# Attention, gated MLP and soft mixture of experts in one kernel: w_outT's loads in two pairs, fold products in fp32r, the last long block's dispatch behind chunk 4, output columns in three parts

## The chip, the cores and the metric

The kernel runs on one core of one Trainium2 chip. The metric is the device time of one execution in microseconds (us); lower is better. Before the change it is 473.82 us, the median of three runs (473.59 to 474.17).

## What is computed

The reference, cut to what matters:

```python
# attention: batch 4, 8 heads, 768 tokens, head dimension 64, chunks of 32 queries
for c in range(nc):
    q_c = q[:, :, c_start:c_end]                       # 32 queries
    k_full = concatenate([mem_k, k[l_start:r_end]])    # 8 memory keys, 16 to the left, 32, 8 to the right
    scores = scale * q_c @ k_full.T; a = softmax(scores)
    out[:, :, c_start:c_end] = a @ v_full
x = out as [3072 tokens, 512]
h = x @ w_in                                           # 512 to 2048
x = (h * sigmoid(h)) @ w_out                           # 2048 to 512
logits = x @ phi                                       # 32 slots, 4 for each of 8 experts
d = softmax(logits, over the tokens); slot_input = d.T @ x
h = maximum(slot_input[e] @ w1[e], 0); slot_out[e] = h @ w2[e]     # 512 to 1024 to 512
return softmax(logits, over the slots) @ slot_out      # [3072, 512]
```

## The kernel before the change

**Units and blocks.** Attention goes by units of 128 tokens, 24 of them. The MLP goes by seven blocks of 2, 4, 4, 4, 4, 4 and 2 units (256, then 512, then 256 tokens); block 0 and the last block, 6, are the short ones. A block has 16 chunks of 128 hidden features (k from 0 to 15). Each chunk (`pe_mlp`, L287 to L303) is 12 TensorE products: x and w_in are each held as a rounded fp32r part and a rest (`wh`, `wl`; x high and low), and three of the four products of these are taken. ACT casts w_in to `wh` (`act_wh`, L444), POOL and once DVE take the rest (`low_part`, L496). After a chunk, ACT takes the tanh (L404), DVE the gate product g (L505) and a 32x32 transpose of it (L515). Chunk c waits on TensorE for g of chunk c-2.

**Attention of a unit.** TensorE: scores (`pe_scores`, L259). DVE: maximum and subtraction (L476, L478). ACT: exp (L424). DVE: sums and reciprocals (`dve_sums`, L485 to L489). POOL: normalising (L776). TensorE: transposes of the probabilities (L268). ACT and DVE copy these to `pt` (L414). TensorE: product with v (`pe_values`, L282). ACT and DVE write x as its two parts (L434, L494). Units 0 and 1 are done ahead of block 0. The units of the next block are woven between the chunks of the present one: `values_at` and `scores_at` (L48 to L57) say which unit has its values and which its scores in each quarter of a block. In block 0 TensorE transposes the probabilities after chunks 1, 5, 9, 13, and has values of unit 2, 3, 4, 5 and then scores of the next unit after chunks 2, 6, 10, 14.

**Logits without the MLP's output.** w_out and phi are multiplied first: `pe_w2` (L340), 16 products (32 records) of phi with w_outT after chunk 13 of block 0, which need all four w_outT loads; they are transposed after chunk 14 (`pe_w2_T`) and copied to `w2c` (L568). The logits of a block come straight from g (`pe_logits`, L316), in four partition groups. `pe_fold` (L324) sums the groups with a 0/1 matrix `fold`, in fp32: DVE copies them to `part` (L519), the fold follows after chunk 2 of the next block. DVE takes the running maximum (L524, L526), ACT the exp (L439), DVE transposes that to `eB` (L531) and the raw logits to `logits` (L536), and updates the running total (L543).

**Dispatch.** `pe_dispatch` (L336) multiplies these weights with g, so that the sum over tokens is taken of g and not of the MLP's output; DVE adds to `acc` with a decay (L546 to L560). `dispatch_step` (L356) puts it behind chunk 4 of the next block, in the last block behind chunk 7. The fold of block 5 uses the bank `lu_ps`, into which the dispatch writes too; that of block 6 uses `pt_ps`.

**Tail.** After block 6: its own logits, fold and dispatch, with dummy products (`keep_busy`, L899) between them; a sum over groups (L928, L932), the product with w_out (L944), the experts' first layer (L964), its second layer `ffn2` (L652) in two halves of 256 columns, the sums over groups (`slot_outputs`, L660), and the combination of slots by token (`outputs`, L687) in six rounds of 1 MB: three for the left half, run between the tiles of the right half's ffn2, and three after it. ACT and DVE copy each round out of PSUM (L815, L895), SyncE stores it.

**Transfers.** All are issued by SyncE, in one written order with waits (L717 to L756): q/k (0.625 MB) and v (0.5 MB) of each unit, in rings of two; w_in, w_outT, w_out, w1, w2 in pieces of 1 MB. From L609 on, `places` says where each of the 36 late pieces goes and what must be over first: 4 of w_out, 16 of w1, 16 of w2. The order begins with

```python
load_qk(0); load_qk(1); load_v(0); load_w_in(0); load_v(1); load_qk(2); load_w_in(1)
load_qk(3); load_v(2); load_w_in(2); load_v(3); load_w_in(3); load_qk(4); load_v(4)
phi; load_wot(0); load_wot(1); load_qk(5); load_v(5); load_wot(2); load_wot(3); load_qk(6); load_v(6)
```

where load_qk(u) waits for the scores of unit u-2, load_v(u) for the values of unit u-2.

Of the kernel before, what the change touches and what calls it, by code (L numbers as in the profile page):

```python
# [7 lines left out]
QT = 64  # L8
# [3 lines left out]
KC = DM // 128  # L12
# [9 lines left out]
SB = 2  # L22
# [42 lines left out]
def by_token(rounds):  # L65

    import numpy as np
    y = np.empty((NT * QT // 128, 128, DM), rounds.dtype)
    tiles = y.reshape(NT, QT, DM)
    for h in range(2):  # L70
        cols = slice(h * 256, (h + 1) * 256)
        for i, (G0, G1) in enumerate(PAIR):
            got = rounds[h * ROUNDS + i].reshape(128, 2, 4, 256).transpose(1, 2, 0, 3)
            y[4 * G0 - 2:4 * G0 + 2, :, cols] = got[0]
            if G1:
                y[4 * G1 - 2:4 * G1 + 2, :, cols] = got[1]
            else:
                tiles[0:4, :, cols] = got[1][:, 0:64]
                tiles[NT - 4:NT, :, cols] = got[1][:, 64:128]
    return y.reshape(NT * QT, DM)  # L80


def moe_program(nc, qk, v, w_in, w_outT, w_out, phi, w1, w2, out):
# [5 lines left out]
    with ExitStack() as ctx:  # L89
# [21 lines left out]
        eB = at("eB", 4096, [128, TMAX])  # L111
        stats = at("stats", 4608, [128, 8])
# [30 lines left out]
        units.append(at("unit_acc", 1536, [128, HALF_W]))  # L143
        phi_sb = part[:, 0:KC * SLOTS].rearrange("p (k s) -> p k s", k=KC)
# [52 lines left out]
        wh_done, wl_first, wl_done = sem("wh_done"), sem("wl_first"), sem("wl_done")  # L197
# [5 lines left out]
        h_mm, tanh_done, g_done, gb_done = sem("h_mm"), sem("tanh_done"), sem("g_done"), sem("gb_done")  # L203
        l_mm, part_done, fold_mm = sem("l_mm"), sem("part_done"), sem("fold_mm")
# [42 lines left out]
        def pe_scores(pe, u, dispatched=0):  # L247
# [5 lines left out]
            for t in range(2):  # L253
                for c in range(2):
                    for p in range(PAIRS):
                        for h2 in range(2):
                            a, r = place_of(p, h2)
                            at = (2 * t + c) * WIN
                            last = nc.tensor.matmul(s_of(u)[32 * r:32 * r + 32, a, at:at + WIN], q_of(u, t, c, p, h2),  # L259
                                                    k_of(u, t, c, p, h2), start=True, stop=True)  # L260
# [26 lines left out]
        def pe_mlp(pe, b, k):  # L287
# [32 lines left out]
        def pe_fold(pe, b):  # L320
# [3 lines left out]
            nc.tensor.matmul(raw_ps(b)[:, 0:TOKS[b]], fold[:], part[:, 0:TOKS[b]], start=True, stop=True).then_inc(fold_mm, 1)  # L324

        def pe_dispatch(pe, b, units_scored):
            pe.wait_ge(et_done, b + 1)
            pe.wait_ge(raw_kept, 4 * min(b + 1, LAST))
# [27 lines left out]
        def dispatch_step(b):  # L356
            return 7 if b == LAST else 4

        def pe_block(pe, b):
            for k in range(NCH):  # L360
# [6 lines left out]
                if b and k == dispatch_step(b):  # L367
# [7 lines left out]
                if b == 0 and k == 13:  # L375
                    pe_w2(pe)
                if at_pause and scores_at(b, n) is not None:
# [661 lines left out]
```

## Time and profile before the change

| | |
|---|---|
| median of 3 runs | 473.82 us (473.59 to 474.17) |
| the profiled execution | 473.49 us |
| its span | 471.7 us |
| granted TensorE clock, mean | 0.996 of full speed |
| TensorE busy | 451.2 us (96%) |
| weight loads busy | 332.6 us (71%) |
| DVE busy | 274.4 us (58%) |
| ACT busy | 138.7 us (29%) |
| POOL busy | 45.3 us (10%) |
| read and written in HBM | 74.51 MB and 6.29 MB |

All times in the rows below count from the start of the span of the profiled execution. A row of the timeline is one or several like instructions: start, duration, engine, line, what it writes and reads, how many, and in brackets the time for which the engine had stood before it and what ended this. "SPq" is SyncE issuing transfers. The share of a transfer stage is a mean over the core's 16 DMA engines. A TensorE product of fp32 data is two records. Products overlap, so the time from one start to the next is what one costs.

### The profile page before, as it was taken

How to read it: one execution, taken by the hardware profiler on the slowest of the kernel's cores; microseconds unless marked ns; L12 is line 12 of the kernel's file. 1: busy time of each engine (PE TensorE's matmuls, PEld its weight loads, DVE VectorE, ACT ScalarE, POOL GpSimd, SP SyncE). 2: the span in 40 equal slices, each digit the busy share in tenths (PEclk: the TensorE clock that was granted, in tenths of full speed). 3: DMA queues.
4: the chain of work that ended last, by engine and by line, in shares of the span. 5: the costliest groups of instructions: out<-in, count | busy, mean ns of one | idle time of the engine just before them, and what ended most of it. 6: DMA issues, size and time to landing. Idle time of an engine off the chain costs nothing.

```text
span 471.7 us, 12280 instructions
## 1 busy us (share of the span) xinstructions
PE 451.2 (96%) x5460; PEld 332.6 (71%) x5460; DVE 274.4 (58%) x532; ACT 138.7 (29%) x255; POOL 45.3 (10%) x43
## 2 busy tenths in 40 slices
PE   5899999999999999999999999999999999999982
PEld 5799667777876787767777777787677778643551
DVE  5657457765586566766665675568544566551233
ACT  2655233232331322323332323323222121210022
POOL 2476000000000000000000000000000000010000
PEclk9999999999999999999999999999999999999998
DMA  8979222321142153303331231130150479999997
GB/s 330 405 295 375 90 95 96 103 92 50 60 191 55 49 190 101 102 1 102 103 96 51 57 101 60 47 131 1 27 243 0 179 263 406 376 401 423 421 423 323
DMA packets 14308, 81.59 MB, mean 173 GB/s; under 512 B 1584, under 2 KB 1712, under 8 KB 7856
## 3 DMA queue, kind: packets, MB, share of 16 engines
q1 hardware_dynamic: 14256, 80.81, 45.4%
q8 instruction: 43, 0.70, 0.6%
q14 instruction: 9, 0.07, 0.0%
HBM read 74.51 MB, written 6.29 MB: 171 GB/s over the span
## 4 chain that ended last, share of the span: by engine, by line
PE 85%; DMA 6%; DVE 4%; ACT 1%; POOL 1%; issue 1%; DVEq 0%; POOLq 0%
PE h_ps L300 55%; PE o_ps L282 6%; DMA unit<-w 5%; PE lpu_ps L316 5%; PE lpu_ps L336 4%; PE sx_ps L259 3%; PE pt_ps L268 2%; PE sx_ps L336 2%; PE h_ps L964 1%; PE sx_ps L901 1%; POOL sc L776 1%; PE lpu_ps L324 1%; PE h_ps L901 1%; DMA qk_sb<-qk 1%; PE o_ps L944 1%
## 5 line engine op out<-in xcount | busy, mean ns | idle before, releaser
L300 PE MATMUL h_ps<-x_odd,wh 128*128 128x512 f32 x384 | 126.8, 400 | 0.0
L505 DVE SCALAR_TENSOR_TENSOR gT<-gT,h_ps 128x512 f32<-128x512 f32 (+1 forms) x108 | 66.4, 615 | 95.5 <-ACT gT L404 95.0
L404 ACT ACTIVATE gT<-h_ps 128x512 f32<-128x512 f32 (+1 forms) x108 | 58.6, 543 | 185.5 <-PE h_ps L300 184.5
L300 PEld LDWEIGHTS h_ps<-x_odd,wh 128*128 128x128 f32 x384 | 72.1, 188 | 21.4 <-issue 5.1
L300 PE MATMUL h_ps<-x_even,wh 128*128 128x512 f32 x256 | 85.0, 400 | 0.0
L300 PE MATMUL h_ps<-x_odd,wl 128*128 128x512 f32 x192 | 74.9, 390 | 0.0
L515 DVE STREAM_TRANSPOSE gB<-gT 128x512 f32<-128x512 f32 x80 | 56.7, 708 | 2.1 <-issue 0.3
L300 PEld LDWEIGHTS h_ps<-x_even,wh 128*128 128x128 f32 x256 | 48.0, 188 | 12.6 <-issue 2.2
L776 POOL TENSOR_TENSOR sc<-sc,row_stats 128x512 f32<-128x512 f32 x23 | 24.0, 1045 | 280.2 <-DVE row_stats L489 280.2
L300 PE MATMUL h_ps<-x_short,wh 128*128 128x256 f32 x256 | 50.6, 290 | 0.3 <-DVE x_short L494 0.3
L300 PE MATMUL h_ps<-x_even,wl 128*128 128x512 f32 x128 | 49.9, 390 | 0.0
L300 PEld LDWEIGHTS h_ps<-x_short,wh 128*128 128x128 f32 x256 | 41.0, 191 | 5.0 <-issue 3.2
L300 PEld LDWEIGHTS h_ps<-x_odd,wl 128*128 128x128 f32 x192 | 36.1, 188 | 7.4 <-issue 0.5
L300 PE MATMUL h_ps<-x_short,wl 128*128 128x256 f32 x128 | 36.2, 282 | 0.0
L282 PEld LDWEIGHTS o_ps<-pt,v_sb 128*64 128x64 f32 x768 | 24.4, 138 | 8.0 <-issue 7.3
L424 ACT ACTIVATE sc<-sc 128x512 f32<-128x512 f32 x23 | 14.5, 631 | 52.5 <-DVE sc L478 52.4
L282 PE MATMUL o_ps<-pt,v_sb 128*64 128x64 f32 x768 | 27.6, 225 | 0.8 <-DVE pt L414 0.8
L414 ACT COPY pt<-pt_ps 64x512 f32<-64x512 f32 x46 | 26.5, 577 | 6.3 <-PE pt_ps L268 5.8
L300 PEld LDWEIGHTS h_ps<-x_even,wl 128*128 128x128 f32 x128 | 24.1, 188 | 5.1 <-issue 0.5
L259 PEld LDWEIGHTS sx_ps<-qk_sb 64*32 64x32 f32 x1472 | 16.3, 107 | 14.8 <-issue 14.0
L300 PEld LDWEIGHTS h_ps<-x_short,wl 128*128 128x128 f32 x128 | 24.4, 191 | 0.3 <-issue 0.2
L316 PE MATMUL lpu_ps<-gT,w2c 128*32 128x512 f32 (+1 forms) x184 | 22.8, 576 | 0.7 <-DVE w2c L568 0.7
(185 smaller groups left out, 495.4 us busy)
## 6 DMA issues: line engine op xcount, KB each, us to landing
unit<-w SPq DMA_DIRECT2D x31, 1024.0 KB, 9.3
qk_sb<-qk SPq DMA_DIRECT2D x24, 640.0 KB, 5.5
v_sb<-v SPq DMA_DIRECT2D x24, 512.0 KB, 3.6
out<-unit SPq DMA_DIRECT2D x6, 1024.0 KB, 7.4
w_stage<-w_in SPq DMA_DIRECT2D x4, 1024.0 KB, 8.0
wot<-w_outT SPq DMA_DIRECT2D x4, 1024.0 KB, 8.8
unit<-w_out SPq DMA_DIRECT2D x4, 1024.0 KB, 5.4
unit_acc<-w SPq DMA_DIRECT2D x1, 1024.0 KB, 10.2
```

The costliest lines, as they stand in the source:

```text
L259: last = nc.tensor.matmul(s_of(u)[32 * r:32 * r + 32, a, at:at + WIN], q_of(u, t, c, p, h2), k_of(u, t, c, p, h2), start=True, stop=True)
L268: last = nc.tensor.transpose(pt_ps[:, j * 128:(j + 1) * 128], sc_u(u)[:, 2 * j:2 * j + 2, :].rearrange("p c k -> p (c k)"), ident[:])
L282: last = nc.tensor.matmul(o_ps[64 * h2:64 * h2 + 64, at:at + QT], v_sb[:, u % V_RING, t, h * D:(h + 1) * D], pt[:, (2 * a + t) * 4 + r, :] ...
L300: last = nc.tensor.matmul(h_ps[k % 2][:, 0:TOKS[b]], w[:, n, kc, q * 128:(q + 1) * 128], x[:, lo, kc, 0:TOKS[b]], start=(kc == 0 and w is ...
L316: last = nc.tensor.matmul(lg_ps(b)[32 * q:32 * q + 32, 0:TOKS[b]], w2c[:, q, 32 * n:32 * n + 32], gt_of(b, 4 * n + q), start=(n == 0), sto ...
L336: last = nc.tensor.matmul(u_ps[i][32 * c:32 * c + 32, :], eB[32 * i:32 * i + 32, 32 * j:32 * j + 32], gb_groups(b, i, j), start=(r == 0), ...
L404: nc.scalar.activation(gt_of(b, k), h_ps[k % 2][:, 0:TOKS[b]], ACT.Tanh, scale=0.5).then_inc(tanh_done, 1)
L414: copy(pt[half, :, c * CHUNK:(c + 1) * CHUNK], pt_ps[half, :].rearrange("p (j q) -> p j q", q=CHUNK)).then_inc(pt_done, 1)
L424: nc.scalar.activation(sc_u(u)[:], sc_u(u)[:], ACT.Exp, scale=D ** -0.5).then_inc(exp_done, 1)
L505: nc.vector.scalar_tensor_tensor(out=gt_of(b, k), in0=gt_of(b, k), scalar=1.0, in1=h_ps[k % 2][:, 0:TOKS[b]], op0=ALU.add, op1=ALU.mult).t ...
L515: nc.vector.transpose(gb_of(b, k), gt_of(b, k)).then_inc(gb_done, 1)
L776: nc.gpsimd.tensor_tensor(p, p, rinv[:, n % SB, :].unsqueeze(2).to_broadcast([128, 2 * PAIRS, WIN]), ALU.mult).then_inc(p_done, 1)
```

## The change

In the beginning: w_in's first load waits for the first q/k load; load_w_in(3) goes ahead of load_v(3); phi and w_outT's first pair go ahead of load_v(4), and w_outT's second pair ahead of load_v(5). The scores of unit 0 come in two halves, with a maximum of each. DVE has unit 0's sums ahead of unit 1's scores; the normalising of unit 1 is halved between POOL and DVE; the DVE's share of w_in's rest goes to POOL; w_in is cast by column halves and not by row halves, so that two chunks need one half. ACT has cast 1 ahead of unit 1's copy, and exp 2 ahead of cast 2. In block 0 the scores go ahead of the values on TensorE and ahead of x on DVE, the sums ahead of g, the exp one chunk earlier; `pe_w2` goes from chunk 13 to 9, its transposes from 14 to 10.

Folds of blocks 0 to 5: DVE writes the logits as a rounded part and a rest, TensorE takes two fp32r products. Block 5's fold goes to `pt_ps`, and its dispatch goes from chunk 7 to 4 of the last block; the three w1 loads that wait for it go ahead of those that wait for chunk 7.

Tail: fewer dummy products; w_out's four tiles are released one by one; the output columns are finished in three parts of 256, 128 and 128, in seven rounds: three of 1 MB, then 1 and 0.5 MB for either part.

```diff
-ROUNDS = NG // 2
-PAIR = [(1, 2), (3, 4), (5, 0)]
+COLS = [slice(0, 256), slice(256, 384), slice(384, 512)]
+ROUNDS = [(0, (1, 2)), (0, (3, 4)), (0, (5, 0)), (1, (1, 2, 3, 4)), (1, (5, 0)), (2, (1, 2, 3, 4)), (2, (5, 0))]
+DISPATCH_STEP = 4
-W_LOW_BEFORE = {2: (0,), 3: (2, 3), 4: (4, 5), 5: (6, 7)}
+W_LOW_BEFORE = {2: (0, 1), 3: (2, 3), 4: (4, 5), 5: (6, 7)}
...
         def raw_ps(b):
-            return pt_ps if b == LAST else lu_ps
+            return pt_ps if b >= LAST - 1 else lu_ps
...
         def pe_probs_T(pe, u):
             pe.wait_ge(p_done, u + 1)
+            if u == 1:
+                pe.wait_ge(p_half, 1)
...
-            if b == 0 and q == 0:
-                if n == 0:
-                    pe.wait_ge(wl_first, 1)
-                pe.wait_ge(wl_done, 2 * n + 1)
+            if b == 0 and q % 2 == 0:
+                pe.wait_ge(wl_done, 2 * n + q // 2 + 1)
...
+            if b == LAST - 1:
+                pe.wait_ge(pt_done, 2 * NUN)
+            if b == LAST:
+                pe.wait_ge(raw_kept, 4 * LAST)
...
+            pe.wait_ge(fold_rounded, 1)
+            nc.tensor.matmul(raw_ps(b)[:, 0:TOKS[b]], fold_r[:], part_hi[:, 0:TOKS[b]], start=True, stop=False)
+            nc.tensor.matmul(raw_ps(b)[:, 0:TOKS[b]], fold_r[:], part_lo[:, 0:TOKS[b]], start=False, stop=True).then_inc(fold_mm, 1)
...
+                if b == 0 and at_pause:
+                    pe_scores(pe, scores_at(0, n))
                 if at_pause and values_at(b, n) is not None:
                     pe_values(pe, values_at(b, n))
...
-                if b == 0 and k == 13:
+                if b == 0 and k == 9:
                     pe_w2(pe)
...
+            nc.vector.tensor_copy(part_hi[:, 0:TOKS[b]], lg_ps(b)[:, 0:TOKS[b]]).then_inc(parthi_done, 1)
+            dve.wait_ge(parthi_done, b + 1)
+            if b:
+                dve.wait_ge(u_mm, b)
+            nc.vector.tensor_tensor(part_lo[:, 0:TOKS[b]], lg_ps(b)[:, 0:TOKS[b]], part_hi[:, 0:TOKS[b]].bitcast(fp32),
+                                    ALU.subtract).then_inc(part_done, 1)
...
-                if b and k % 4 == pause(b) + 1 and scores_at(b, n) is not None:
+                if k % 4 == pause(b) + 1 and scores_at(b, n) is not None:
                     dve_sums(dve, scores_at(b, n))
...
-            if n == 1:
+            if n == 0:
                 places += [(i, u_mm, NB - 1) for i in (9, 10, 11)]
...
-        places += [(places[u][0], si_mm, 1) for u in range(NF)]
+        places += [(places[u][0], si_mm, u + 1) for u in range(NF)]
...
             load_v(0)
+            sp.wait_ge(qk_in[0], 16)
             load_w_in(0)
...
             load_w_in(2)
+            load_w_in(3)
             load_v(3)
-            load_w_in(3)
             load_qk(4)
-            load_v(4)
             sp.dma_start(phi_sb, phi).then_inc(phi_in, 16)
             load_wot(0)
             load_wot(1)
+            load_v(4)
             load_qk(5)
-            load_v(5)
             load_wot(2)
             load_wot(3)
+            load_v(5)
...
             act_wh(act, 0)
             act_x(act, 0)
+            act_wh(act, 1)
             act_pt(act, 1)
-            act_wh(act, 1)
             act_x(act, 1)
+            act_exp(act, 2)
             act_wh(act, 2)
-            act_exp(act, 2)
...
-            dve_scores(dve, 0)
-            dve_scores(dve, 1)
-            dve_sums(dve, 0)
-            dve_sums(dve, 1)
-            pt_half(dve, nc.vector.tensor_copy, 0, 1)
...
+            dve_first_scores(dve)
+            dve_sums(dve, 0)
+            dve_scores(dve, 1)
+            pt_half(dve, nc.vector.tensor_copy, 0, 1)
+            dve_sums(dve, 1)
+            normalise(nc.vector, dve, 1, 4, 2 * PAIRS, p_half)
             dve_x(dve, 0)
             pt_half(dve, nc.vector.tensor_copy, 1, 1)
-            low_part(nc.vector, dve, 1, wl_first)
+            dve_scores(dve, 2)
             dve_x(dve, 1)
-            dve_scores(dve, 2)
...
-            for e in range(E):
-                ffn2(pe, 1, e)
-                if e == 0:
-                    slot_outputs(pe, 0)
-                if e % 2 and e // 2 < ROUNDS:
-                    outputs(pe, 0, e // 2)
-            keep_busy(3, ex_ps)
-            slot_outputs(pe, 1)
-            keep_busy(4, ex_ps)
-            for i in range(ROUNDS):
-                outputs(pe, 1, i)
+            for part in (1, 2):
+                for e in range(E):
+                    ffn2(pe, part, e)
+                    if e == 0:
+                        slot_outputs(pe, part - 1)
+                    if e % 2 and part == 1 and e < 6:
+                        outputs(pe, e // 2)
+                    if part == 2 and e in (1, 3):
+                        outputs(pe, 3 + e // 2)
+            keep_busy(3, s_ps)
+            slot_outputs(pe, 2)
+            keep_busy(4, s_ps)
+            outputs(pe, 5)
+            outputs(pe, 6)
```

## Rows read from the trace of the kernel before

**Rows 1.** Busy time by stage: from:to, length, PE, PEld, DVE, ACT, POOL, clock, DMA share, GB/s

```profile
196.00:260.00 64.00, 64.00 (x758) 47.79 (x758) 41.23 (x73) 19.86 (x36) 4.18 (x4) 1.00 0.26 77
...
384.00:386.00 2.00, 1.76 (x39) 1.39 (x42) 1.64 (x5) 0.59 (x2) 0.00 (x0) 1.00 0.58 246
...
462.00:464.00 2.00, 1.15 (x16) 0.77 (x16) 1.84 (x4) 1.42 (x4) 0.00 (x0) 1.00 0.57 238
468.00:470.00 2.00, 0.00 (x0) 0.00 (x0) 0.00 (x0) 0.00 (x0) 0.00 (x0) 0.50 1.06 442
```

**Rows 2.** Timeline of the beginning: units 0 and 1, first MLP chunk, unit 2

```profile
7.58 0.63 ACT L424 ACTIVATE sc<-sc 128x512 f32<-128x512 f32 x1 [5.56 <-DVE sc L478]
...
9.23 0.68 DVE L485 TENSOR_REDUCE row_stats<-sc 128x8 f32<-128x512 f32 x1
...
10.50 1.04 POOL L776 TENSOR_TENSOR sc<-sc,row_stats 128x512 f32<-128x512 f32 x1 [7.26 <-DVE row_stats L489]
...
19.01 0.39 PE L300 MATMUL h_ps<-x_short,wh 128*128 128x256 f32 x1 [0.31 <-DVE x_short L494]
...
23.28 0.66 PE L268 MATMUL pt_ps<-ident,sc 128*128 128x128 f32 x4 [1.14 <-POOL sc L776]
```

**Rows 3.** Timeline of block 0: transposes of units 3 and 5, the first logits

```profile
32.14 0.66 PE L268 MATMUL pt_ps<-ident,sc 128*128 128x128 f32 x4 [0.41 <-POOL sc L776]
...
50.07 0.66 PE L268 MATMUL pt_ps<-ident,sc 128*128 128x128 f32 x4 [0.60 <-POOL sc L776]
...
60.56 1.50 PE L316 MATMUL lpu_ps<-gT,w2c 128*32 128x256 f32 x24 [0.75 <-DVE w2c L568]
```

**Rows 4.** The chain that ended last: start, duration, engine, tile, line, records

```profile
50.73 3.57 PE lpu_ps L346 x32
...
134.44 0.86 PE lpu_ps L324 x2
135.30 5.49 PE h_ps L300 x24
```

**Rows 5.** Issues of q/k 4 and of w_outT 2 and 3, us to landing

```profile
18.49 0.43 SPq L704 DMA_DIRECT2D qk_sb<-qk  x1
...
qk_sb<-qk SPq DMA_DIRECT2D x1, 640.0 KB, 9.1
...
35.72 0.92 SPq L715 DMA_DIRECT2D wot<-w_outT  x2
...
wot<-w_outT SPq DMA_DIRECT2D x1, 1024.0 KB, 8.0
```

**Rows 6.** Timeline of block 2: the running total, then the dispatch

```profile
139.43 0.22 DVE L543 SCALAR_TENSOR_TENSOR stats<-stats 128x1 f32<-128x1 f32 x1
...
141.16 0.61 PE L336 MATMUL lpu_ps<-gB,eB 32*32 32x512 f32 x1
```

**Rows 7.** The tail: issues and chunks in time, each issue's us to landing

```profile
385.25 0.33 SPq L743 DMA_DIRECT2D unit<-w  x1
...
389.91 3.07 PE h_ps L300 x24
...
403.16 0.33 SPq L743 DMA_DIRECT2D unit<-w  x1
...
unit<-w SPq DMA_DIRECT2D x1, 1024.0 KB, 7.1
...
431.71 24.93 DMA unit<-w
...
462.45 0.33 SPq L755 DMA_DIRECT2D out<-unit  x1
...
out<-unit SPq DMA_DIRECT2D x1, 1024.0 KB, 4.0
...
465.09 0.33 SPq L755 DMA_DIRECT2D out<-unit  x1
...
out<-unit SPq DMA_DIRECT2D x1, 1024.0 KB, 6.2
```

More of the change, by code:

```diff
@@ L62, in pause, with width, words, by_token @@
     return 2 if b == 0 else 1
-def by_token(rounds):
+def width(r):
+    return COLS[ROUNDS[r][0]].stop - COLS[ROUNDS[r][0]].start
+def words(r):
+    return 4 * len(ROUNDS[r][1]) * width(r)
+def by_token(stored):
     import numpy as np
-    y = np.empty((NT * QT // 128, 128, DM), rounds.dtype)
+    y = np.empty((NT * QT // 128, 128, DM), stored.dtype)
     tiles = y.reshape(NT, QT, DM)
[L70 to L76, printed above, removed]
-            else:
-                tiles[0:4, :, cols] = got[1][:, 0:64]
-                tiles[NT - 4:NT, :, cols] = got[1][:, 64:128]
+    for r, (part, groups) in enumerate(ROUNDS):
+        sixth, at = STORED[r]
+        cols = COLS[part]
+        got = stored[sixth][:, at:at + words(r)].reshape(128, len(groups), 4, width(r)).transpose(1, 2, 0, 3)
+        for rows, G in zip(got, groups):
+            if G:
+                y[4 * G - 2:4 * G + 2, :, cols] = rows
+            else:
+                tiles[0:4, :, cols] = rows[:, 0:64]
+                tiles[NT - 4:NT, :, cols] = rows[:, 64:128]
     return y.reshape(NT * QT, DM)
@@ L252, in pe_scores @@
                 pe.wait_ge(acc_done, 4 * dispatched - 1)
[L253 to L260, printed above, removed]
+            for ps in (range(0, 2), range(2, 4)) if u == 0 else (range(PAIRS),):
+                if ps[0]:
+                    last.then_inc(s_first, 1)
+                for t, c, p, h2 in itertools.product(range(2), range(2), ps, range(2)):
+                    a, r = place_of(p, h2)
+                    at = (2 * t + c) * WIN
+                    last = nc.tensor.matmul(s_of(u)[32 * r:32 * r + 32, a, at:at + WIN], q_of(u, t, c, p, h2),
+                                            k_of(u, t, c, p, h2), start=True, stop=True)
             last.then_inc(s_mm, 1)
@@ L621, in moe_program @@
         sources += [w1[4 * q + j, i] for q in range(2) for i in range(2) for j in range(4)]
-        sources += [w2[h, e] for h in range(2) for e in range(E)]
+        sources += [w2[i] for i in range(2 * E)]
         out_u = [units[places[NF + u][0]] for u in range(NU - own - NF, 2 * E)]
@@ L669, in out_ps, with slot_outputs @@
-        def out_ps(r):
-            return out_sets[1 if r > ROUNDS and (r - ROUNDS) % 2 else 0]
-        def outputs(pe, h, i):
-            r = ROUNDS * h + i
-            if i == 0:
-                pe.wait_ge(so_done, h + 1)
-                if h == 0:
-                    pe.wait_ge(cT_done, 1)
-            before = r if r <= ROUNDS else r - 1
-            if before:
-                pe.wait_ge(out_act, 2 * before)
-                pe.wait_ge(out_dve, 2 * before)
-            for gg in range(2):
+        def slot_outputs(pe, part):
+            n = COLS[part].stop - COLS[part].start
+            pe.wait_ge(so_cp, part + 1)
+            nc.tensor.matmul(so_ps[part][:, 0:n], fold[:], so_in[:, COLS[part]], start=True, stop=True).then_inc(so_mm, 1)
@@ new lines, in dve_slot_outputs, with outputs @@
+        def dve_slot_outputs(dve, part):
+            n = COLS[part].stop - COLS[part].start
+            dve.wait_ge(ffn2_mm, part + 1)
+            nc.vector.tensor_copy(so_in[:, COLS[part]], ffn2_ps[part][:, 0:n]).then_inc(so_cp, 1)
+            dve.wait_ge(so_mm, part + 1)
+            nc.vector.tensor_copy(so4[:, COLS[part]], so_ps[part][:, 0:n]).then_inc(so_done, 1)
+        def out_ps(r):
+            return out_sets[r == NR - 1]
+        def outputs(pe, r):
+            part, groups = ROUNDS[r]
+            n = width(r)
+            if r == 0:
+                pe.wait_ge(cT_done, 1)
+            pe.wait_ge(so_done, part + 1)
+            others = r - 1 if r == NR - 1 else r
+            if others:
+                pe.wait_ge(out_act, 2 * others)
+                pe.wait_ge(out_dve, 2 * others)
+            for i, G in enumerate(groups):
@@ L782, in _ @@
         def _(act):
+            act.wait_ge(const_set, 5)
+            nc.scalar.copy(fold_r[:], fold[:]).then_inc(fold_rounded, 1)
             act_exp(act, 0)
```

163 lines of the change are left out of this document (91 added, 72 removed).

## Prediction

> **What bounds the kernel now.** I read the table of stages first. In blocks 1 to 5 TensorE is busy without a gap (64.00 of 64.00 us) and DVE is at 41.23 [rows 1]: there only TensorE's own work counts. In block 0 TensorE stands once per attention unit, waiting for the normalised probabilities: 1.14 us before unit 2, 0.41 before unit 3 (the gap before unit 4 is like it), 0.60 before unit 5, and 0.75 for w2c at the end [rows 2, 3]. From chunk 15 of the last block on the transfers bound. The load issued behind that chunk, at 403.16, lands 7.1 us later, at 410.3, and the last load, 18 loads on, at 431.71 + 24.93 = 456.64: 2.57 us each. The last of the six stores is down 14.65 us after that (465.09 + 6.2 = 471.3): 2.44 us each [rows 7]. So one transfer of 1 MB follows another to the end, and only an earlier start of this queue, or fewer bytes, would shorten it. The change moves the same bytes.
>
> **The parts, against the profiled execution.** Its time is 473.49 us (span 471.7); the median of the three runs is 0.33 us above it.
>
> A. *First MLP chunk.* Unit 0's exp starts at 7.58 and takes 0.63, but its sums start only at 9.23, behind unit 1's scores, and the normalising follows at 10.50 [rows 2]. With sums 0 ahead they start at about 8.0 (0.3 us of it from the scores in halves), so unit 0 gains 1.2 us. Unit 1's chain now starts behind sums 0, which costs about 1.2; halving its normalising between DVE and POOL gives back up to half of 1.04, and its wait behind unit 0 on TensorE was 1.1 anyway. On ACT the cast of w_in's second half now stands ahead of unit 1's copy, and with the scores of unit 2 on DVE x of unit 1 comes out 0.8 us earlier: chunk 0 starts at 18.2, not 19.0. Gain 0.8; ends 0 (DVE's order gives nothing) and 1.2. w_in's first load waits for the first q/k load; I cost that at nothing, since the two transfers ahead of it still keep the queue full until it could start.
>
> B. *Unit 2.* Exp 2 now comes ahead of a cast, its scores ahead of x of unit 1. Its normalising is done about 20.4, and TensorE gets there at 18.2 + 3.0 = 21.2 instead of 22.1. The 1.14 us stall [rows 2] goes: 1.1 (0.6 to 1.1).
>
> C. *Rounds of units 3 and 4.* Scores go ahead of values, which takes about 1.1 us out of the loop; but the sums now stand ahead of g of the same chunk, and two chunks later TensorE waits for that g, by my count 0.3 of the 0.5 gained. I take 0.3 of each round's gap, 0.6 for both (0 to 0.9). TensorE then comes to the transposes of unit 4 at 41.0 - 0.8 - 1.1 - 0.6 = 38.5.
>
> D. *w2's product at chunk 9 instead of 13.* Its work, 3.57 us [rows 4], is only moved. But it needs all four w_outT loads, at 38.5 + 0.5 = 39.0. Now the third of them lands at 35.72 + 8.0 = 43.7 [rows 5], and the fourth one transfer later, at 46.2. The new order issues the first two before unit 2's values, at about 19, and the last two at about 26, behind v 4 and q/k 5. The queue is full until q/k 4 lands, at 18.49 + 9.1 = 27.6 [rows 5]. Behind that come, by size, 5.1 transfers of 1 MB: four of w_outT, v 4 (0.5) and q/k 5 (0.625). At 2.57 us [rows 7] these are 13.2, and I add an estimated 0.7 for phi's many small rows: 41.5. So TensorE, which had no wait here, stands 2.5 us: cost 2.5. Ends: 0 (all in time) and 7.2 (landing as late as now, 46.2). I take 2.5: the spacing of queued transfers is the nearest row.
>
> E. *Rest of block 0.* w2c is ready long before the logits, so the 0.75 goes; of the 0.60 before unit 5 [rows 3] a part stays, behind g as in C, and the transposing of w2 moves with its copy on DVE. Gain 1.1 (0.6 to 1.4).
>
> Block 0 together: 0.8 + 1.1 + 0.6 - 2.5 + 1.1 = 1.1 us.
>
> F. *Folds.* A fold of 512 columns in two fp32 passes takes 0.86; 24 products of fp32r take 5.49, 0.23 each [rows 4]. Two of them are 0.46: 0.40 less. Four such folds lie in blocks 2 to 5, one of 256 columns in block 1 (0.2): 1.8 us, all on TensorE's path. The second DVE operation (0.7) sits in front of the transposes of e and of the raw logits; what follows these on DVE, the running total, starts at 139.43 while the dispatch starts at 141.16 [rows 6]: 1.7 us of slack for 0.7, and 0.4 for TensorE's earlier coming, so nothing. The fifth 512 fold, in block 6, has chunks half as long ahead of it, and DVE's second operation eats a part: counted in G. Ends 1.2 and 2.0.
>
> G. *Tail.* The dispatch of block 5 ends about 384.1 instead of 389.9 (after it 24 products begin at 389.91), and the three loads that hang on it now go ahead of the pair issued at 385.25 [rows 7]. Before that pair the queue has a hole: the DMA share is 0.58 in 384 to 386 [rows 1]. With loads issued at 384.1 the queue runs about 1.2 us earlier. But the load behind chunk 15 cannot start before that chunk ends, and this moves only by the fold's 0.3; the 7.1 us that the load now takes are 3.1 more than the 4.0 of a store that finds the queue free (462.45) [rows 7], so it still stands in a queue, and what the queue gains counts. Net 1.2; ends 0.3 and 2.5. Fewer dummy products, si's four separate releases and DVE's earlier adding to acc save time on TensorE, but none on the queue, which is still full when their loads come: nothing.
>
> H. *Three parts at the end.* Only 1.5 of 6 MB of stores are left after the last load's outputs instead of 3. By the mean share of the DMA engines (0.57 in 462 to 464 [rows 1], and the slice before is like it) some 1.7 us between 460 and 464 are empty and could be filled. The Trainium skill (DMA: Bandwidth & Descriptors, Queues, rings and completion order) says that one copy is split over up to 16 engines, each of which consumes its own ring in order: then a lagging engine sets the landing, and idle ones cannot help it. By the mean share the sum would be 1.7 us better, by that rule nothing. The landings decide for me: six stores in 14.65 us are the full pace, with no hole [rows 7]. So 0 (up to 1.7). The extra 128 small weight loads, the seventh store and the pairs of experts per load lie under the transfers: nothing, and 0.5 if that cover were gone.
>
> Sum: 1.1 + 1.8 + 1.2 = 4.1 us; 473.5 becomes 469.4, and from the median 473.8 becomes **469.7**.
>
> **Rivals.** *w_outT in time.* If the transfers go faster than the spacings say, D is nothing: 467.2. Against it: 13 us of queued bytes behind the landing at 27.6. For it: the two ends of a transfer's pace, 2.44 and 2.57, differ by only 0.7 over five, so it takes a TensorE later than 38.5 at unit 4 too. Chance 0.2.
>
> *The end is filled.* The mean share is right, H gives 1.7: 468.0. For it: the share of 0.57; against it, the pace of the stores. Chance 0.2.
>
> *The queue does not start earlier.* The loads behind chunk 15 set it again, G is 0.3: 470.6. Chance 0.14.
>
> *Slower: w_outT lands as late as now.* The place is w2's product at chunk 9. If the fourth load lands at 46.2, the wait is 7.2 instead of 2.5: 474.4. It also leaves TensorE idle so long that its clock may fall, as at the end, where its last products end before 464 and the granted clock is 0.50 in 468 to 470, the 1.2 GHz level [rows 1]. The Trainium skill (TensorE: Matmul & The Clock Gate, What's actually happening) has the same: an idle array is gated to half rate until it has been busy again. Every us of product work at that level costs one more; with 3 of them the time is 477. It decides from a wait of 2.5 + 4.1 = 6.6 us, a landing at 45.6. Against it: nothing in the new order holds the last two issues beyond unit 2's values. Chance 0.06.
>
> The forecast itself has 0.4. A measurement of this kernel can tell about 0.2% (0.95 us) from no change. Faster by more, below 472.9: 0.90, all cases but the slow one, less 0.04 for a wait in D of over 5.5 us, which gives no change: 0.04; slower: 0.06. The range reaches from both good rivals together (467.2 - 1.2) to D at 5 us: 466.0 to 472.3.
>
> **What would show it.** Chunk 0 of block 0 at about 18.2; no gap before unit 2; a wait for w_outT of about 2.5 us in the first w2 product near 39; block 1's first chunk 1.1 us earlier; the folds at 0.46; block 5's dispatch right behind chunk 4 of the last block; stores still 2.45 us apart to the end. I am wrong if TensorE waits for g or the halved unit 1 longer than counted, if w_outT is there, or if the last load lands less than 14.5 us before the end.

## Result, and the profile after

The changed kernel takes 471.09 us (median of 19 runs, 469.67 to 473.03). The kernel before, beside it on the same chip, takes 473.9 us (19 runs, 472.92 to 474.93). The ratio is 0.9936, 95% interval 0.9925 to 0.9947: faster by 0.64%, where 469.7 us was forecast with a range from 466.0 to 472.3. The profiled execution takes 471.36 us with a span of 469.4, so 2.3 us less than the one before (471.7); the forecast's sum was 4.1. One execution of experiment 2, which took 734.23 us at a granted clock of 0.561, is left out of its median as a slow one.

The table of stages of the kernel after, with the columns of [rows 1]:

```profile
196.00:260.00 64.00, 64.00 (x761) 48.21 (x760) 42.08 (x75) 20.23 (x37) 4.18 (x4) 1.00 0.26 80
384.00:386.00 2.00, 2.00 (x20) 1.91 (x17) 1.86 (x5) 0.19 (x2) 0.00 (x0) 1.00 0.97 406
462.00:464.00 2.00, 0.85 (x32) 0.65 (x24) 1.53 (x3) 1.53 (x4) 0.00 (x0) 1.00 0.38 143
468.00:470.00 2.00, 0.00 (x0) 0.00 (x0) 0.00 (x0) 0.00 (x0) 0.00 (x0) 0.50 0.23 90
```

The middle is as before. The transfers' queue is full at 384 (0.97, was 0.58), as G wanted, but between 462 and 464 it is emptier than before (0.38, was 0.57). The hole near the end was there before too and has moved with the rest: over the whole hole the mean shares leave 1.7 us of 460 to 464 empty before, and 1.9 us of 461 to 465 after.

The beginning and block 0 of the kernel after, from the timeline, the lines that answer to [rows 2, 3]:

```profile
8.43 0.69 DVE L526 TENSOR_REDUCE row_stats<-sc 128x8 f32<-128x512 f32 x1 [0.70 <-ACT sc L453]
9.71 1.04 POOL L536 TENSOR_TENSOR sc<-sc,row_stats 128x512 f32<-128x512 f32 x1 [6.48 <-DVE row_stats L530]
13.39 0.42 DVE L536 TENSOR_TENSOR sc_first<-sc_first,row_stats 128x256 f32<-128x256 f32 x1
13.43 0.85 POOL L536 TENSOR_TENSOR sc_first<-sc_first,row_stats 128x256 f32<-128x256 f32 x1 [2.68 <-DVE row_stats L530]
18.46 0.38 PE L321 MATMUL h_ps<-x_short,wh 128*128 128x256 f32 x1 [0.32 <-DVE x_short L542]
21.43 0.60 PE L291 MATMUL pt_ps<-ident,sc 128*128 128x128 f32 x4
38.42 0.60 PE L291 MATMUL pt_ps<-ident,sc 128*128 128x128 f32 x4
40.28 1.05 PE L376 MATMUL lpu_ps<-wot,part 128*32 128x512 f32 x2 [0.28 <-DMA wot<-w_outT]
42.75 3.62 PE L376 MATMUL lpu_ps<-wot,part 128*32 128x512 f32 x26 [1.42 <-DMA wot<-w_outT]
60.50 1.50 PE L337 MATMUL lpu_ps<-gT,w2c 128*32 128x256 f32 x24
```

Chunk 0 starts at 18.46 (was 19.01), the waits for the probabilities are gone (2.6 us in all before), and unit 4's transposes stand at 38.42, where the forecast had 38.5. Then TensorE is in w2's product from 38.95 to 46.37, 7.42 us for 3.57 of work [rows 4]: 3.85 us of waiting, at a product that did not wait before. The chain of waits tells how much of the gain it takes (start, duration, what):

```profile
26.99 15.71 DMA wot<-w_outT
42.75 3.62 PE lpu_ps L376 x26
...
62.00 2.96 PE h_ps L321 x12
...
322.70 0.23 PE lpu_ps L353
322.92 0.23 PE lpu_ps L354
...
389.20 1.70 PE h_ps L321 x12
...
397.98 3.07 PE h_ps L321 x24
...
455.99 1.22 PE lpu_ps L710 x38
457.22 1.06 issue
458.28 1.03 PE lpu_ps L710 x26
```

Block 1's first chunk stands at 62.00, 0.06 us earlier than before (62.06): block 0's gains are all given back. The last 24 products of the MLP, chunks 14 and 15 of the last block, start at 397.98 (before 400.06), the last store has landed at 468.98 (471.31). So by stage: block 0 gains 0.06, blocks 1 to 6 up to those products gain 2.02 (338.00 becomes 335.98), and the tail, from those products to the last store, gains 0.25 (71.25 becomes 71.00). In the chain of the tail a transfer no longer stands, as it did before with 24.93 us [rows 7]; products, copies out of PSUM and 1.06 us of "issue" do.

### The profile page after: what moved, and what is told of

Its sections match the earlier page's. It is cut to its first block, busy times and chain, and to the rows that moved or that the text cites. A ratio compares the mean times of both kernels' runs of the same rounds, so it can differ in the third digit from the quotient of the medians.

```text
span 469.4 us, 12642 instructions
## 1 busy us (share of the span) xinstructions
PE 451.4 (96%) x5626; PEld 336.0 (72%) x5626; DVE 277.5 (59%) x544; ACT 139.0 (30%) x258; POOL 47.4 (10%) x44
## 4 chain that ended last, share of the span: by engine, by line
PE 88%; DMA 6%; DVE 3%; issue 1%; ACT 0%; SPq 0%; DVEq 0%
PE h_ps L321 54%; PE o_ps L305 5%; PE lpu_ps L337 5%; PE sx_ps L280 4%; PE lpu_ps L366 4%; DMA wot<-w_outT 3%; DMA qk_sb<-qk 3%; PE lpu_ps L710 2%; PE sx_ps L366 2%; PE pt_ps L291 2%; PE h_ps L1024 2%; DVE unit L955 1%; PE h_ps L745 1%; PE sx_ps L961 1%; PE o_ps L1004 1%
## 5 line engine op out<-in xcount | busy, mean ns | idle before, releaser
L280 PEld LDWEIGHTS sx_ps<-qk_sb 64*32 64x32 f32 x1472 | 16.6, 107 | 15.2 <-issue 13.8
```

## The experiments

"At 11" below is the changed kernel with w2's product two chunks later, "after" the changed kernel itself, and "run 5" is experiment 5. Readings of the profiles, in us of the span. The landings are those of the trace's completion records; where two are given, they are the first and the last of the 16 DMA engines. "Product" is the start of the last 26 records of w2's product (at 11: of all 32; before: of all 32 too), "chunk 14" that of the last 24 products of the MLP (chunks 14 and 15 of the last block), "experts" the end of the last expert's product.

```
                        product  block 1  chunk 14  last load        experts  last store  chunk 14 to last store
before                   50.73    62.06    400.06   453.62 456.64    457.75   471.31      71.25
after                    42.75    62.00    397.98   450.76 452.88    459.31   468.98      71.00
w2 at 11                 43.76    57.69    393.66   445.88 448.29    455.40   465.07      71.41
fp32 folds               42.41    61.67    399.89   452.94 456.86    461.51   471.53      71.64
two halves               41.33    60.58    396.56   449.38 453.12    455.09   471.03      74.47
dispatch at 7            42.31    61.55    397.06   450.48 453.32    458.32   467.99      70.93
at 11, round 4 later                       393.87   446.78 449.01    455.58   466.83      72.96
at 11, two halves                 57.77    393.76   445.99 449.04    450.15   465.62      71.86
at 11, dispatch at 7              57.93    393.58   446.43 450.09    455.32   464.99      71.41
at 11, shifted                             394.31   447.27 450.14    458.09   467.74      73.43
at 11, round 4 last               57.69    393.80   446.41 449.47    454.46   465.70      71.90
unit 1 whole             42.86    62.12    398.10   451.34 453.71    459.65   469.31      71.21
scores 0 whole           41.48    60.76    396.87   449.40 452.54    458.21   467.87      71.00
sums 0 late              42.06    61.32    397.42   450.30 453.09    458.89   468.55      71.13
```

**1. w2's product behind chunk 11.**

The same in TensorE's order and in DVE's:

```diff
-if b == 0 and k == 9:
+if b == 0 and k == 11:
...
-if b == 0 and k == 10:
+if b == 0 and k == 12:
```

> w2's product moves from chunk 9 to 11 of block 0 (its transposes to 12), nothing else. Theory: at chunk 9 TensorE stands about 3.8 us for w_outT (product from 38.95 to 46.37 in the changed kernel, 3.57 of it work), and at chunk 11 it would come at about 43.8, after the last landing at 42.7: no wait, block 1's first chunk near 58.5 instead of 62.0, time 471.1 - 3.5 = 467.6. Rival: the wait only stands in for one that follows anyway (w2c late, attention of unit 5 late): block 1 starts at 61 to 62, time 470 to 471.

467.54 us (6 runs), ratio to before 0.9879 (0.9858 to 0.9901). The chain:

```profile
40.34 0.79 PE sx_ps L280 x53
...
43.83 3.57 PE lpu_ps L376 x32
...
57.69 2.96 PE h_ps L321 x12
```

The product takes its 3.57 us in one piece and block 1 starts 4.31 us earlier than after; the medians of the two differ by 3.6 us. Of the 4.31, 3.85 are the wait and 0.12 an earlier chunk 0 (18.34); the remaining 0.34 is not broken down. The rival, that another wait takes its place, falls. That the landing itself sets block 1's start shows in the seven profiles with the product at 9: from the product's last 26 records to block 1 it is 19.24 to 19.28 us in each, while the start itself moves between 60.58 and 62.12 with the landing.

**2. fp32 folds.** All folds again one fp32 product of `part`, DVE's rounding and subtraction left out.

```diff
-nc.tensor.matmul(raw_ps(b)[:, 0:TOKS[b]], fold_r[:], part_hi[:, 0:TOKS[b]], start=True, stop=False)
-nc.tensor.matmul(raw_ps(b)[:, 0:TOKS[b]], fold_r[:], part_lo[:, 0:TOKS[b]], start=False, stop=True).then_inc(fold_mm, 1)
+nc.tensor.matmul(raw_ps(b)[:, 0:TOKS[b]], fold[:], part[:, 0:TOKS[b]], start=True, stop=True).then_inc(fold_mm, 1)
```

> The folds of blocks 0 to 5 are fp32 again and DVE writes one copy; order and banks stay as changed. Theory: TensorE's path gives back 0.4 us for each of five long folds and 0.2 for the short one, 2.2 us: 473.3. Rival: DVE's second operation and its waits cost as much as the faster product gains, then 471.1 to 471.6.

472.91 us (11 runs), ratio 0.9989 (0.9974 to 1.0003). Blocks 1 to 6 take 338.22 instead of 335.98: the folds are worth 2.24 us, and are nearly all that the change as it stands brings.

**3. Two halves.** COLS, ROUNDS and the order behind the second ffn as before.

```diff
-COLS = [slice(0, 256), slice(256, 384), slice(384, 512)]
+COLS = [slice(0, 256), slice(256, 512)]
```

> Output columns in two halves again (six rounds of 1 MB, w2 laid out in halves), all else as changed. Theory: in the changed kernel the end hangs on TensorE and the copies out of PSUM (last load down at 452.9, last store 16.1 us later, where the queue alone needs 14.7); with halves the last store comes 14.7 us after the last load again: 469.6. Rival: the three parts did fill the queue at the end, and halves cost up to 1.7 more: 472.8.

469.99 us (10 runs), ratio 0.9939 (0.9919 to 0.9958), against 0.9936 (0.9925 to 0.9947) of the three parts: no difference that can be told. Its profiled execution is its slowest (473.42, mean clock 0.987), so its 74.47 us of tail are not its usual ones; the other runs lie between 469.26 and 472.13. TensorE waits 2.42 us for the last load in it, the granted clock is 0.50 from 452.81 to 456.22, and the last 16 records of the experts take 1.93 us where they took 1.07 before. The theory's 469.6 holds as a number, the rival's 472.8 does not: three parts bring nothing over two halves. The theory's mechanism, a last store 14.7 us behind the last load, is not what this profile shows (17.9).

**4. Dispatch of block 5 behind chunk 7**, DVE's adding to acc and the three loads with it.

```diff
-if b and k == DISPATCH_STEP:
+if b and k == (7 if b == LAST else DISPATCH_STEP):
```

> Block 5's dispatch behind chunk 7 of the last block again, its three loads behind chunk 7's pair; all else as changed. Theory: the queue starts 1.2 to 1.5 us later and the last load lands at about 454.4, but the end hangs on TensorE and the copies, and TensorE loses the stall behind DVE's adding to acc (0.5): 470.6 to 471.2. Rival: the queue still sets the end, then 472.4.

470.46 us (6 runs), ratio 0.9933 (0.9913 to 0.9953): not slower than the change. From block 1 to chunk 14 it takes 335.51 instead of 335.98, and the tail is as long (70.93 and 71.00), though the last load lands 56.26 us behind chunk 14 instead of 54.90. That difference of 1.4 is one pair of executions: in the eleven profiles with the dispatch at 4 the load lands 54.6 to 57.0 us behind chunk 14, median 55.7, in the three with it at 7 (before, runs 4 and 7) 56.3 to 56.6. So the early dispatch gives the queue some 0.8 us, and the end gets none of it.

**5 to 7. The same ends on the faster beginning.** Each is "at 11" and one part of the tail more: the fifth round of outputs behind expert 5 instead of 3; two halves; the dispatch behind chunk 7.

> w2's product behind chunk 11, and of the three-part ending the fifth round of outputs issued behind expert 5 instead of expert 3. Theory (TensorE and the copies out of PSUM set the end now: 0.49 us of the wait for VectorE's copies in front of the fifth round goes, as two experts' products fill it): the last load to the last store 16.3 us where the kernel with the product at 11 alone has 16.8, time 467.0. Rival (the stores set the end, 2.45 us apart): nothing changes, 467.5. If the hole of 1.5 us in the last experts' products (its idle time has the label issue) belongs to its place among TensorE's instructions, it stays in the same product; if it belongs to a moment, it moves.

> w2's product behind chunk 11 and the ending in two halves as in the kernel before. Theory (all stores stand behind all loads in one queue, so both endings have the same floor, 6 MB at 2.45 us per MB = 14.7 us behind the last load, and the halves reach it where TensorE is not held up): last load near 448.5, last store near 463.5, time 465.5 to 466.5. Rival (TensorE's wait for the last load lets its clock fall, as in the profile of the halves with the product at 9): last store 17 to 18 us behind the last load, 467.5 to 469.

> w2's product behind chunk 11 and the last long block's dispatch behind chunk 7 as before. Theory (the earlier dispatch only trades a wait for g against the loads' start): the three loads are issued about 5 us later, the last load lands 0 to 1.2 us later than 448.5, time 467.5 to 468.7. Rival (the dispatch at 4 costs TensorE more than it gives the queue, as the run with the dispatch at 7 and the product at 9 hinted with 470.46 against 471.09): 466.9.

468.22 us (6 runs; ratio 0.988, 0.9861 to 0.99), 468.01 (5 runs; 0.9874, 0.9855 to 0.9894) and 467.38 (4 runs; 0.9857, 0.9839 to 0.9875). The three intervals overlap each other's and that of "at 11". Run 5 gained nothing. Its profiled execution has a tail 1.55 us longer than that of "at 11", and nearly all of it is clock: TensorE stands 1.86 us from 452.69 on, the granted clock is 0.50 from 455.86 to 459.27, and the sum over groups with the idle products around it takes 3.42 us instead of 1.97. Three of its runs had no such fall in their mean clock (0.997) and took 467.29 to 467.46, as "at 11". Run 6 shows the halves' other side: the experts are done at 450.15, 5.2 us earlier than with three parts, but 3 MB of stores follow instead of 1.5, and the last store lands 16.6 us behind the last load, not 14.7. Its theory's end of 463.5 is missed, but the rival's reason is not there either: the granted clock stays at 1.00 until 458.56, behind TensorE's last product. The fourth store is issued at 454.85, 5.8 us behind the last load as before the change; its first engine is done 3.7 us later, as before, its last one 5.9 us later, where it was 4.0. One late engine costs these 1.9 us. Run 7 has its last load 1.8 us later than "at 11" and its last store 0.1 us earlier: a load that comes earlier or later by that much changed nothing there. Its 467.38 lies between its theory and its rival, and the intervals decide for neither.

**8. Sixteen more idle products** behind the last product of ffn 1's second half, "at 11" else.

```diff
+if q == 1 and kc == 3:
+    keep_busy(16, s_ps)
```

> w2's product behind chunk 11, and 16 more idle products of 128 columns (64 more instructions on TensorE) behind the last product of the second ffn's first layer, where TensorE waits for loads anyway. Theory (the hole of 1.0 to 1.5 us in the last experts' products is TensorE waiting for its own instructions, whose 16 KB packets stand behind the bulk loads and stores in the same DMA engines): the hole lies 32 products earlier in TensorE's order, at or ahead of the first products of expert 4 of the last part, and ends about 1.4 us behind the end of an instruction packet, as in the three profiles that show it; time 466.5 to 468. Rival (it belongs to this place: a bank, a unit, a semaphore): it stays in expert 6's products, time 467.5 plus what the added products cost, up to 2.

470.04 us (5 runs), ratio 0.9914 (0.99 to 0.9928): 2.5 us slower than "at 11" for 3.8 us of added products, beyond what the theory had. It assumed that TensorE had room there, and TensorE has none: the experts end 2.7 us later (458.09 for 455.40). The hole is gone:

```profile
454.04 1.30 DVE unit L955 x2
456.20 1.88 PE lpu_ps L710 x64
```

Expert 6's products are there, without it, so the rival (a bank, a unit, a semaphore of this place) falls. The theory wanted the hole ahead of expert 4's first products; there TensorE waits for the copies and arrives 2.5 us behind the end of the packet of instructions at 453.74. So the run agrees with the theory and does not show it by itself. Run 11 does more.

**9, 10 and 12. The beginning's parts**, each undone alone in the changed kernel: unit 1 normalised by POOL alone; unit 0's scores in one run with both maxima behind them; sums 0 behind the scores of unit 1.

```diff
-dve_sums(dve, 0)
 dve_scores(dve, 1)
+dve_sums(dve, 0)
```

> The changed kernel with unit 1 normalised whole on GpSimd as before, all else kept; read at the first chunk of the MLP, which stands at 18.46 (18.2 to 18.5 in the other profiles). Theory (the two halves run at the same time on VectorE and GpSimd and hold each other up: GpSimd's half takes 0.85 us of the whole's 1.04): the first chunk only 0.2 us later, 18.65. Rival (the halving is what gained the 0.55): 19.0. Time within 0.5 us of 471.1 in either case, since w2's product waits for w_outT.

> The changed kernel with VectorE's two maxima of unit 0 both behind its last score; TensorE's scores in one run in the old order. Read at VectorE's sums of unit 0 (8.43 now, 9.23 in the kernel before) and at the first chunk (18.46). Theory (the first chunk's 0.55 us come from unit 0 being ready earlier): the sums at 8.8 to 8.9 and the first chunk at 18.8 to 18.9. Rival (behind unit 0 stands another wait, for unit 1 or for a transfer): the sums later, the first chunk still at 18.4 to 18.5. Time within 0.5 us of 471.1 in either case.

> The changed kernel with VectorE's sums of unit 0 put back behind its scores of unit 1, all else kept. Theory (of the beginning's parts this order alone gained at the first chunk; the halves of unit 0's scores gave nothing and those of unit 1's normalising 0.12): the sums at 9.2 to 9.4, the first chunk at 18.9 to 19.1 instead of 18.34 to 18.58. Rival (unit 1's chain, not unit 0's, sets the first chunk): the sums at 9.3, the first chunk at 18.2 to 18.5. In either case w2's product still waits for w_outT, whose last load has landed at 41.3 to 42.9 in the profiles so far, and the time is 470 to 472.

471.69, 470.26 and 470.93 us, one run each: the runs of the changed kernel alone lie between 469.67 and 473.03, so these times tell nothing, and the places in the profiles are what is read. The first chunk, from the timelines of the three in this order:

```profile
18.58 0.39 PE L319 MATMUL h_ps<-x_short,wh 128*128 128x256 f32 x1 [0.32 <-DVE x_short L540]
```

```profile
18.41 0.39 PE L319 MATMUL h_ps<-x_short,wh 128*128 128x256 f32 x1 [0.31 <-DVE x_short L540]
```

```profile
9.93 0.68 DVE L526 TENSOR_REDUCE row_stats<-sc 128x8 f32<-128x512 f32 x1
...
19.87 0.39 PE L321 MATMUL h_ps<-x_short,wh 128*128 128x256 f32 x1 [0.31 <-DVE x_short L542]
```

Undoing the halved normalising costs 0.12 us and undoing the halved scores gains 0.05, both less than the spread of the first chunk in the ten profiles with an unchanged beginning (18.23 to 18.58): no effect that can be told. Unit 0's scores take 1.18 us whole and 1.54 in halves, which eats what the earlier first maximum gains; its sums start at 8.45 with the scores whole and at 8.43 in halves. The order of the sums is worth 1.3 to 1.6, more than the 0.55 to 0.75 expected, since without it the new rest of the beginning is slower than the old (19.87 for 19.01). And yet run 12, whose chunk 0 starts 1.41 us later than after, starts block 1 0.68 us earlier: its w_outT landed earlier. What is gained ahead of w2's product is spent in its wait.

**11. The fifth round of outputs behind the last expert**, in place of three idle products, with DVE's copy of the last part's sums ahead of that round's copies; "at 11" else.

```diff
-if part == 2 and e in (1, 3):
-    outputs(pe, 3 + e // 2)
-keep_busy(3, s_ps)
+if part == 2 and e == 1:
+    outputs(pe, 3)
+outputs(pe, 4)
```

> w2's product behind chunk 11, and the fifth round of outputs behind the last expert's products in place of three idle ones, with VectorE's copy of the last part's products ahead of its copies of that round. Theory (TensorE is the bound from chunk 15 to the last ffn's end, 455.4 with the last load in at 448.5, and the hole with the label issue is its wait for its own instructions): the last ffn ends 1.3 to 1.5 us earlier, the sixth round starts 0.5 to 0.9 us earlier, last store 15.9 to 16.3 us behind the last load; the hole stands one round (24 to 32 products) later in the order of the code, ahead of or in the fifth round; time 466.6 to 467.2. Rival (the copies out of PSUM set the end): the last ffn earlier but the sixth round no earlier, 467.5 to 468.

467.99 us (4 runs), ratio 0.9864 (0.9844 to 0.9885): no faster than "at 11". The experts end 0.94 us earlier, not 1.3 to 1.5, but the sixth round starts at 457.23 where it was 457.32. The idle products in front of it and its own products run at half pace, in the chains of "at 11" and then of this run:

```profile
456.49 0.89 PE sx_ps L961 x8
```

```profile
455.58 1.72 PE sx_ps L967 x8
457.30 0.51 PE h_ps L745 x2
```

The granted clock is 0.50 from 455.36 to 458.77 here, behind a stand of 1.84 us, and stays at 1.00 to 463.57 in "at 11". It costs 0.8 us in the idle products and 0.7 in the sixth round. DVE had stood 3.05 us when it began its copies of that round, so the rival, that the copies set the end, is not shown either. What the order would give at the full clock stays open: the other three runs, with a mean clock of 0.995 to 0.997, took 466.62, 467.92 and 468.07. The hole has moved. The last experts' products in the timeline of "at 11", and then of this run:

```profile
449.35 1.08 PE L710 MATMUL lpu_ps<-unit,gT 128*32 128x128 f32 x32
451.58 1.29 PE L710 MATMUL lpu_ps<-unit,gT 128*32 128x128 f32 x38
454.37 1.03 PE L710 MATMUL lpu_ps<-unit,gT 128*32 128x128 f32 x26 [1.50 <-issue]
```

```profile
449.50 2.60 PE L710 MATMUL lpu_ps<-unit,gT 128*32 128x128 f32 x87
453.94 0.52 PE L710 MATMUL lpu_ps<-unit,gT 128*32 128x128 f32 x9 [1.84 <-issue]
```

It stood in the middle of expert 6 (70 of 96 records done), where no wait is written, and now stands 17 records later. The round taken away in front of it is 8 products, 16 records. So the hole keeps its place in the count of TensorE's instructions, whatever code is there: 5536 or 5537 products and 5664 or 5665 weight loads lie ahead of it in each of the ten profiles that have it. With the packets of instructions that the trace lists in the DMA engines (16384 bytes each):

```
                        packet           TensorE resumes   behind the packet's end
after                   455.83 - 456.85  458.28            1.43
w2 at 11                451.84 - 452.86  454.37            1.51
dispatch at 7           454.85 - 455.84  457.29            1.45
at 11, round 4 later    452.26 - 453.30  454.55            1.25
at 11, dispatch at 7    451.94 - 452.96  454.29            1.33
at 11, round 4 last     451.62 - 452.66  453.94            1.28
```

Runs 2, 9, 10 and 12 have the hole at the same record (38 or 39 of 64) and resume 1.59, 1.26, 1.40 and 1.40 us behind a packet's end. The Trainium skill (Advanced Engine Details and Errata, ISA Cache) gives an instruction cache with lines of 16 KB, 256 instructions. The packets have that size, and a cache that runs dry is what both facts look like, but no run shows that it is one. No run made the hole go away for nothing, so what its 1.0 to 1.9 us cost at the end, and why the packet comes so late, stays open. It costs more than itself in two of the ten profiles: those with the longest holes, 1.84 and 1.86 us, are those in which the clock fell behind it, while TensorE still had products to run.

## Why the prediction was right and where it was not

The sign, the range and the kind of most effects hold; the sum was 1.8 us too good (4.1 for 2.3), by 1.0 in block 0 and by 0.95 in the tail, with 0.2 back in the blocks between.

**A, first chunk.** Forecast 0.8, measured 0.55, and 0.43 to 0.78 in the ten profiles with this beginning. The mechanism is the order of the sums, as said (run 12). The halves were counted too high: 0.3 us for the scores and up to 0.5 for the normalising, where neither shows an effect beyond the spread. There POOL's half takes 0.85 us beside DVE's 0.42, where half of 1.04 is 0.52: had it begun only when DVE's half ended (13.39 + 0.42 = 13.81), it would end at 14.33, and it ends at 14.28. The Trainium skill (SBUF — State Buffer, Who interferes with whom) says just this: a DVE instruction with two inputs in SBUF and a GpSimd instruction that reads SBUF exclude each other, the later one for the whole of the other. The trace agrees.

**B, C, E, the stalls.** Right: no gap before unit 2 or 4, unit 4 at 38.42 for 38.5. The waits before unit 5 and for w2c (0.60 and 0.75) are gone too.

**D, the wait for w_outT.** The mechanism and its place were right, its size was not: 3.85 us for 2.5. The last load landed at 42.70, not 41.5, and TensorE came at 38.95 as forecast. It is one landing of many: in the thirteen profiles with this order of loads the last one is down between 41.16 and 42.82, so 41.5 lies among them. In the six of them in which TensorE comes to the product at 38.7 to 39.6, its wait is 2.6 to 3.85 us, and the one shown here is the longest. What failed is "the spacing of queued transfers is the nearest row": the landing is that of the slowest of 16 engines, and the spread between them differs from one execution to the next. By the trace's completion records the first engine had finished that load at 38.66, before TensorE asked for it, and the last at 42.70. In the seven profiles with the product at 9 it resumes between 41.33 and 42.86, and block 1 follows it to 0.04 us. The rule of the Trainium skill that the prediction cited for H (DMA: Bandwidth & Descriptors, Queues, rings and completion order), that each engine works through its own ring in order, fits this: a row's landing says when the last of them came. The wait also takes what A, B, C and E gain around it: without the wait block 0 gains 4.37 us (62.06 to 57.69) where A, B, C and E were put at 3.6, with it 0.06 where 1.1 was forecast. The rival "w_outT in time", 467.2 us, is what run 1 made of the kernel (467.54), by moving the product instead of the loads.

**F, folds.** 0.46 us each, as forecast; in all 2.24 (run 2), for 1.8 here and the 0.3 of block 5's fold that was counted in G.

**G, the queue's start.** Its mechanism holds: last load 3.76 us earlier, of which 2.08 are the earlier chunk 14 and 1.7 the queue's (forecast 1.2; by the medians under run 4 some 0.8). But the end gets nearly nothing of it, and its price was left out. Behind the early dispatch TensorE now waits for g, which stands on DVE behind the transposes of the raw logits and two additions to acc, as the chain between 383 and 389 has it:

```profile
384.71 0.31 DVE logits L592
385.05 0.45 DVE gB_short L563
385.53 0.61 DVE acc L610
...
387.94 0.61 DVE acc L610
...
388.81 0.34 DVE gT L553
...
389.20 1.70 PE h_ps L321 x12
```

Runs 4 and 7 give 0.5 and 0.3 us for it (335.98 against 335.51 from block 1 to chunk 14, 335.97 against 335.65). The rival "the queue does not start earlier" names the right size for the wrong reason: it does start earlier, and another resource ends the kernel.

**H, three parts.** The step that failed is "lie under the transfers: nothing, and 0.5 if that cover were gone". The cover is gone. Before, the last expert's product ended 1.1 us behind the last load, and the last store landed 14.67 us behind that load, six transfers at 2.45. Now the experts end 6.4 us behind the last load (459.31 against 452.88): 1.5 us of waits for the copies out of PSUM, the hole of 1.06, and two rounds of outputs that stand ahead of them. In eight of the nine profiles that keep this order with a mean clock of 0.996 or more (after, runs 1, 4, 7 to 10 and 12) the last store lands 9.65 to 9.67 us behind the end of the experts, while from the last load it is 14.7 to 17.6. In the ninth, run 2, it is 10.02 from the experts and 14.67 from the last load. So there are two floors, and the later one sets the end: the last load plus 14.67, or the experts plus 9.66, which are 4.52 of TensorE and copies to the sixth issue, 3.96 for its 1 MB to land and 1.19 for the last half. Run 2 stands on the first, run 4 on both, and the changed kernel on the second, 1.4 us above the first: that is how G's 1.7 us are lost, and the tail is 0.25 us shorter where 1.2 was forecast. The halves have the opposite fault, 3 MB behind the last expert, and come out alike. The rival "the end is filled" falls: the mean shares from 461 to 465 (0.85, 0.64, 0.12 and 0.48 of each us) leave 1.9 us empty, and those from 460 to 464 before (0.74, 0.45, 0.25 and 0.88) left 1.7. The first engine is done with the fifth store at 462.47, and the sixth is issued only at 463.83.

Nothing supports the slower rival: w_outT did not land at 46.2 and the clock in 36 to 45 stayed at 1.00.

In short: 471.09 us is 473.9 less some 2.2 of folds and 0.6 of all the rest; with w2's product two chunks later the rest is worth some 3.5 us more (467.54). That kernel, and the same with the dispatch at 7 (467.38, ratio 0.9857), beat both.

## What to carry to other kernels

A consumer that is moved to where its loads land "just about" takes the spread of 16 engines as its wait, and that wait swallows every gain ahead of it; put it behind the latest landing seen, not the mean, as long as its result has slack. Before an end is cut finer, ask what bounds it when the transfers come earlier: the transfers' floor and TensorE's path lay here within 1.4 us of each other in the changed kernel, so more rounds, more instructions and one more wait took all that the queue had gained. And undo each part alone: of this change only the folds paid, and the beginning's parts would have, had one product not waited for them all. Read the granted clock of the stretch, too, before a profile is taken for the usual execution: three of the experiments' profiles had it at half for 3.41 us while TensorE still worked, and their tails were some 1.4 to 1.5 us longer for it.

## What was not expected of the hardware

- TensorE stood 1.0 to 1.9 us with nothing to wait for, at the same count of its instructions in ten profiles, and went on 1.25 to 1.6 us behind a 16 KB packet of instructions. It was seen in a stretch of short products that had become the critical path beside a full transfer queue.
- One 1 MB load can be done on its first engine 4.0 us before its last (w_outT 3: 38.66 and 42.70); before the change the same load had 44.24 and 46.17. Why one engine lags was not tried.
- Two halves of one elementwise operation, started 0.04 to 0.05 us apart on DVE and POOL, took 0.42 and 0.85 us in each of the twelve profiles that have them; whole on POOL it takes 1.04.
